# Two routed expert layers: gates gathered as a column of the rows, results scaled as they leave PSUM, choices combined by one addition, last block stored by halves

## The reference

```python
# 1. local attention: each token is a softmax-weighted sum of itself and 6 before it
out = np.einsum('bshk,bskhg->bshg', softmax(weight_gen), x_unf)     # 8 heads, 7 taps

# 2. first expert layer, two of eight experts per token
noisy = x @ w_gate + np.log1p(np.exp(x @ w_noise)) * noise
top2_w = softmax of the two largest
out[mask] += top2_w[mask, k, None] * (np.maximum(x[mask] @ w1[e], 0.0) @ w2[e])

# 3. second expert layer, one of eight
logits = (x / (|x| + 1e-6)) @ (emb / (|emb| + 1e-6)).T / tau
gate_w = softmax(logits) at the argmax
out[mask] = gate_w[mask, None] * (np.maximum(x[mask] @ v1[e], 0.0) @ v2[e])
```

## Time and profile before

| | us |
|---|---|
| runs, median (lowest to highest) | 1224.87 (1224.33 to 1225.34) |
| profiled execution, its own time | 1223.82 |
| its span | 1222.1 |
| PE busy | 1095.9 (90%) |
| DVE busy | 744.1 (61%) |
| ACT busy | 553.1 (45%) |
| POOL busy | 523.2 (43%) |

### The profile page before, as it was taken

The page is one execution under the profiler, slowest core; times in us unless marked ns, Lnnn a source line. Parts: engine busy times, 40 slices in busy tenths (PEclk is TensorE's granted clock), DMA queues, the critical chain, the costliest instruction groups (busy, mean ns, idle before and its releaser), DMA issues.

```text
span 1222.1 us, 27227 instructions
## 1 busy us (share of the span) xinstructions
PE 1095.9 (90%) x8052; PEld 1039.5 (85%) x8052; DVE 744.1 (61%) x1406; ACT 553.1 (45%) x1552; POOL 523.2 (43%) x639
## 2 busy tenths in 40 slices
PE   1989188999999999999999999786389999999997
PEld 0556176999999999999999999765279999999997
DVE  8998795446464644646455465386854664466663
ACT  2222285445454544545444454355644554455552
POOL 5887002444444444444444444400324444444444
PEclk9999589999999999999999999988589999999999
DMA  9111201213131121313113111182622313124521
GB/s 325 70 63 52 73 1 42 77 42 99 39 101 42 55 83 40 98 40 101 43 39 93 39 41 41 38 268 92 240 62 64 98 42 100 39 65 125 138 61 35
DMA packets 51188, 97.89 MB, mean 80 GB/s; under 512 B 9651, under 2 KB 33051, under 8 KB 50876
## 3 DMA queue, kind: packets, MB, share of 16 engines
q1 hardware_dynamic: 33084, 61.77, 16.7%
q0 software_dynamic: 18048, 35.42, 10.1%
HBM read 69.62 MB, written 29.10 MB: 81 GB/s over the span
## 4 chain that ended last, share of the span: by engine, by line
PE 78%; DVE 12%; issue 3%; POOL 3%; ACT 2%; DMA 2%; DVEq 0%; POOLq 0%; ACTq 0%; SPq 0%
PE banks L624 22%; PE banks L626 11%; PE banks L610 9%; PE banks L616 7%; PE banks L615 7%; PE banks L611 7%; PE banks L612 7%; DVE prods L889 3%; POOL prods L443 2%; PE banks L586 2%; PE banks L594 2%; PE banks L595 2%; PE banks L550 1%; DVE choices L1092 1%; PE banks L540 1%
## 5 line engine op out<-in xcount | busy, mean ns | idle before, releaser
L1050 DVE SCALAR_TENSOR_TENSOR h_lo<-banks,h_hi 128x256 fp32r<-128x256 f32 x736 | 312.1, 424 | 372.4 <-ACT h_hi L774 315.0
L774 ACT ACTIVATE h_hi<-banks 128x256 fp32r<-128x256 f32 x736 | 283.3, 385 | 448.7 <-PE banks L616 347.6
L624 PE MATMUL banks<-w_hl,h_hi 128*128 128x384 f32 x1472 | 466.0, 353 | 0.0
L626 PE MATMUL banks<-w_hl,h_lo 128*128 128x192 f32 x1472 | 371.1, 252 | 0.0
L626 PEld LDWEIGHTS banks<-w_hl,h_lo 128*128 128x128 f32 x1472 | 279.6, 190 | 0.0
L624 PEld LDWEIGHTS banks<-w_hl,h_hi 128*128 128x128 f32 x1472 | 276.0, 188 | 0.4
L451 POOL DMA_INDIRECT x_slots<-token_rows,gather_idx x192 | 192.4, 1002 | 105.4 <-POOL gather_idx L448 76.2
L610 PE MATMUL banks<-x_hi_a,w_hi 128*128 (+1 forms) x736 | 225.0, 306 | 1.8 <-DVE x_hl_b L1018 1.7
L611 PE MATMUL banks<-x_hi_a,w_lo 128*128 (+1 forms) x736 | 206.5, 281 | 0.0
L616 PE MATMUL banks<-x_hl_b,w_lo 128*128 (+1 forms) x736 | 206.3, 280 | 0.0
L615 PE MATMUL banks<-x_hl_b,w_hi 128*128 (+1 forms) x736 | 205.8, 280 | 0.0
(11 more groups left out here) (170 smaller groups left out, 1255.3 us busy)
## 6 DMA issues: line engine op xcount, KB each, us to landing
raw<-in_moe_w SPq DMA_DIRECT2D x17, 768.0 KB
choices<-choice_rows SPq DMA_DIRECT2D x28, 384.0 KB, 4.2
raw<-in_moe_w SPq DMA_DIRECT2D x17, 512.0 KB
raw<-in_moe_w SPq DMA_DIRECT2D x34, 256.0 KB
x_halo<-in_x SPq DMA_DIRECT2D x2, 2688.0 KB, 15.1
token_rows<-stage SPq DMA_DIRECT2D x14, 384.0 KB, 2.3
token_rows<-rows SPq DMA_DIRECT2D x14, 384.0 KB, 3.9
x_slots<-token_rows,gather_idx POOLq DMA_INDIRECT x192
```

The costliest lines, as they stand in the source:

```text
L624: mm(y[:, i, 0:2 * D], h_hi[:, c % HBUFS, t], w2_hl[u][:, c, :, :], start=c == 0, stop=False)
L626: ins = mm(y[:, i, 0:D], h_lo[:, c % HBUFS, t], w2_hl[u][:, c, 0, :], start=False, stop=c == FC - 1)
L774: sc.activation(h_hi[:, c % HBUFS, :], banks[:, c % HBANKS, 0:BLOCK], ACT.Relu).then_inc(h_hi_ready[m], 1)
L1050: v.scalar_tensor_tensor(h_lo[:, c % HBUFS, :], banks[:, c % HBANKS, 0:BLOCK], 0.0, h_hi[:, c % HBUFS, :].bitcast(F32), ALU.max, ALU.subtr ...
```

## The change

- Rows in DRAM are 193 long (`ROW`); the last value is the gate. `token_rows[0]` now has a copy per choice (14336 rows), so each attention group is stored twice, and `choice_rows` is unchanged. `store_gates` writes the column: four DMAs of 3584 values in the first layer (two choices, two batches), two in the second, each value 4 bytes at a step of 772. The first gather waits for them.
- POOL takes the gates of a block out of the gathered rows to a ring of four (`take_gates`); ACT scales one half of the results by them (`take_half`), DVE multiplies and adds the other (`add_half`), each in two pieces.
- The combination is one addition per group. The rows of the second layer are stored unscaled, after all choices have been loaded. No `keep_clock` per group; 26 idle matmuls ahead of the groups in place of 9, not waiting for the first choice. There are two buffers of turned rows.
- The second router picks on raw scores; 1/tau is in the embeddings, and the norm enters only in the gate. Gates are computed partly while PE ranks, partly before the fourth group of hots. The block table is written after the hots; `positions` is shorter; indices of the first layer point into the doubled rows directly.
- In the last block POOL copies the indices ahead, PE signals the first half (`half_done`), and each half is scaled, added and stored by itself.

```diff
 SP
+                for k in range(CHOICES[0]):
+                    sp.dma_start(token_view(token_rows[0][k * N:(k + 1) * N])[b, :, jj * GROUP:(jj + 1) * GROUP, 0:D],
+                                 stage[g % 2][:]).then_inc(rows_stored[g % 2], 16)
+            def store_gates(m):
+                for k in range(CHOICES[m]):
+                    for b in range(B):
+                        sp.dma_start(token_view(token_rows[m][k * N:(k + 1) * N])[b, :, :, D:D + 1],
+                                     gate[k][:, b * J:(b + 1) * J].unsqueeze(2), allow_slow_non_contiguous=True).then_inc(gates_stored[m], 16)
+            sp.wait_ge(weights_ready, 1)
+            load_expert(w1, w2, 1)
+            sp.wait_ge(gates_ready[0], 1)
+            store_gates(0)
+            with sp.Fori(2, E) as e:
...
+            for g in range(NG):
+                b, jj = divmod(g, GB)
+                sp.wait_ge(rows_ready[1], g + 1)
+                sp.dma_start(token_view(token_rows[1])[b, :, jj * GROUP:(jj + 1) * GROUP, 0:D],
+                             rows[:, g * GROUP:(g + 1) * GROUP, :]).then_inc(x1_stored, 16)
+            sp.wait_ge(gates_ready[1], 1)
+            store_gates(1)
 POOL
+                def take_gates(n):
+                    at = n % RING * HALVES
+                    gp.tensor_copy(gate_ring[:, bass.ds(at if isinstance(n, int) else pool.snap(at), HALVES)].unsqueeze(2),
+                                   x_slots[:, :, D:D + 1]).then_inc(gates_taken[m], 1)
...
                     pool.wait_ge(x_turned[m], g + 3)
+                    take_gates(g + 2)
                     gather(g + 3)
+                    pool.wait_ge(gates_taken[m], g + 3)
...
+                    if last:
+                        pool.wait_ge(stored[m], g * 32)
+                        copy_idx()
+                        pool.wait_ge(idx_copied[m], g * 2 + 4)
+                        pool.wait_ge(half_ready[m], 1)
+                        store_half(0)
+                        pool.wait_ge(y_ready[m], g + 3)
+                        store_half(1)
+                        return
-            for g in range(SCALE_ACT, NG):
-                tiles = slice(g * GROUP, (g + 1) * GROUP)
-                gp.tensor_tensor(rows[:, tiles, :], rows[:, tiles, :],
-                                 gate[0][:, tiles].unsqueeze(2).to_broadcast([P, GROUP, D]), ALU.mult).then_inc(pool_gated, 1)
+            mixture(1, out, N - 1, [(x1_stored, 16 * NG), (gates_stored[1], 16 * B)])
 PE
+                        if last and i == 0:
+                            ins.then_inc(half_done[m], 1)
-            pe.wait_ge(choices_in[0][0], 16)
-            keep_clock(9)
+            keep_clock(26)
-                keep_clock(4)
 ACT
-                    sc.copy(y_half(parity(act, g)), y[:, :, D:2 * D]).then_inc(y_copied[m], 1)
+                    if last and i == 0:
+                        act.wait_ge(half_done[m], 1)
+                    else:
+                        act.wait_ge(h_used[m], g * FC + (FC + HBUFS))
+                    sc.activation(y_half(parity(act, g), i), y[:, i, D:2 * D], ACT.Copy,
+                                  scale=slot_gate(act, g, i)).then_inc(y_copied[m], 1)
-            sc.sqrt(table_probe[:], ident[:, 0:1])
-            with act.Fori(0, SCALE_ACT) as g:
...
 DVE
+                step(v.tensor_tensor_scan(cum[:, 1:], flat, flat, 0.0, ALU.add, ALU.max))
+                first_of_expert, last_of_expert = cum[:, 0:E * T:T], cum[:, T::T]
+                step(v.tensor_tensor(totals[:], last_of_expert, first_of_expert, ALU.subtract))
...
+                    if g == HOT_BUFS:
+                        finish_gates()
...
+                block_table()
                 v.memset(gather_rows[:, cols:cols + AHEAD], 0)
                 dve.wait_ge(hots_used[m], n // ONEHOTS)
...
-                    v.tensor_tensor(slots, y[:, :, 0:D], slots, ALU.add).then_inc(y_ready[m], 1)
+                    ins = v.scalar_tensor_tensor(slots, y[:, i, 0:D], slot_gate(dve, g, i), slots, ALU.mult, ALU.add)
+            for g in range(NG):
+                dve.wait_ge(choices_in[g % CHOICE_BUFS], g // CHOICE_BUFS * 32 + 32)
+                first, second = (choices[g % CHOICE_BUFS][:, k, :].rearrange("p (i d) -> p i d", d=D) for k in range(2))
+                v.tensor_tensor(rows[:, g * GROUP:(g + 1) * GROUP, :], first, second, ALU.add).then_inc(rows_ready[1], 1)
+            def weigh_best():
+                dve.wait_ge(roots_ready, 1)
+                step(v.tensor_scalar(inv_norm[:], inv_norm[:], 1e-6, None, ALU.add))
+                step(v.reciprocal(inv_norm[:], inv_norm[:]))
+                step(v.tensor_tensor(r["noisy"][:], scores, best[0][:].unsqueeze(2).to_broadcast([P, T, E]), ALU.subtract))
+                v.tensor_tensor(r["noisy"][:], r["noisy"][:], inv_norm[:].unsqueeze(2).to_broadcast([P, T, E]),
+                                ALU.mult).then_inc(route_ask[1], 1)
```

More of the change, by code:

```diff
@@ L397, in _ @@
             gp.memset(ident[:], 0.0).then_inc(consts_step, 1)
-            gp.memset(before[:], 1.0).then_inc(consts_step, 1)
+            gp.memset(not_after[:], 0.0).then_inc(consts_step, 1)
             gp.memset(ones[:], 1.0)
@@ L838, in _ @@
             sc.activation(r["noisy"][:], r["noisy"][:], ACT.Exp).then_inc(route_act[1], 1)
-            act.wait_ge(route_ask[1], 2)
-            with act.Fori(0, SCALE_ACT) as g:
-                for i in range(GROUP):
-                    tile = rows[:, bass.ds(g * GROUP + i, 1), :].rearrange("p o d -> p (o d)")
-                    ins = sc.activation(tile, tile, ACT.Copy, scale=gate[0][:, bass.ds(g * GROUP + i, 1)])
-                ins.then_inc(gated, 1)
             hot_rows(1)
@@ L922, in _ @@
             finish_rows(NG - 1)
+            v.memset(cum[:, 0:1], 0.0)
+            step(v.memset(block_end[:, 0:1], 0.0))
             def pick(k, scores):
```

240 lines of the change are left out of this document (119 added, 121 removed).

## The result

The changed kernel takes 1212.58 us (median of 5 runs, 1212.21 to 1213.03), the kernel before 1225.34 beside it (5 runs, 1224.33 to 1226.58): a ratio of 0.9895 [0.9881, 0.9908]. It is 12.8 us faster, where 32.9 were forecast. The profiled execution took 1213.03, its span is 1211.2 (before 1222.1).

A forecast was written before the change was run, and what follows sets the result against it. TensorE bounds the expert blocks; only the mostly-DVE stretches between could shrink. 3.5 + 4.0 + 17.6 + 9.1 - 1.3 = 32.9 us off 1223.82, plus 1.05 for the median, gives 1192; range 1186 to 1198, with rivals 1184 to 1213.

The forecast's parts named there:

- Combination: Adding the two choices, up to the second routing's maximum: 19.6 us earlier, 17.6 without the 2.0 counted at the last block.
- TensorE takes the bound, 2.40: Combination, per group: six transposes 0.99 plus twelve products 1.41 make TensorE the limit, 2.40 us for each of 14 groups.
- Rival 2: Combination: TensorE's clock drops without the clock-keeping matmuls, 3.0 us a group, 1200 in all; chance 0.12, shared with Rival 4.
- The last block: End of each mixture: storing by halves, with indices copied ahead, ends 2.0 us earlier, twice, 4.0 in all.
- the sign: End of the program: the last store would begin about 2.1 us after ACT starts on the last results, 4.1 before.
- The gate column: Both routings: 4-byte gate writes to DRAM stay hidden before the gather, with 36 and 29 ns a write available; zero cost.
- end long before the gather: Second routing: stores of the rows, 5.4 MB, follow the last choice load and finish well ahead of the gather.
- Second routing: From the maximum to POOL's index copy: 32.5 us in place of 41.6, 9.1 less.
- Rival 4: Second routing: small steps stay slow although POOL is idle, 7 us, 1199 in all; chance 0.12, shared with Rival 2.
- First routing: First layer's routing: shorter DVE gate, count and id steps, less gate steps in the hots loop, net 3.5 us earlier.
- Inside the blocks: Expert blocks: extra gate copies and split ACT and DVE steps mostly hidden behind TensorE, 1.3 us lost in all.
- Rival 3: Gate column: 4-byte writes go out one behind another, 1279 at 98.7 ns each, whole gain gone at 58; chance 0.11.

The follow-up runs named there:

- e6: e1 with two clock-keeping matmuls per combination group in place of four; 1199.95 us.
- e1: Changed kernel with the combination's clock-keeping matmuls put back, nine once the first choices have landed and four per group; 1201.44 us.
- e3: Kernel before the change, with only the four clock-keeping matmuls per combination group taken out; 1231.03 us.
- e2: Changed kernel with twenty more clock-keeping matmuls behind the wait for the first choices, none in the groups; 1212.35 us.
- e8: Changed kernel with each mixture's last block back in its old order, waiting for both halves before the stores; 1214.48 us.
- e4: Changed kernel with POOL's copy of the last block's store indices moved ahead of its wait for the previous block's stores; 1211.28 us.
- e10: e6 with the second mixture's table at a row pitch of 832 bytes in place of 772; 1192.07 us.
- e9: e6 with the second mixture's rows widened by POOL and stored in one piece by SP; 1201.51 us.
- e7: Changed kernel with every gate column stored four times, three to unread spare tensors, gathers waiting for all; 1294.63 us.
- e11: e9 with e4's order and 24 in place of 10 clock-keeping matmuls ahead of both mixtures' first turns; 1201.20 us.
- e12: e10 with e4's order and 20 in place of 10 clock-keeping matmuls ahead of the first mixture's first turn; 1190.69 us.

## Why the prediction was wrong

- **Combination, the failed step.** "TensorE takes the bound, 2.40": the two terms, 0.99 and 1.41, were read at a granted clock of 1.00, which the four matmuls held that the same edit removes. Measured without them: 3.73 at 0.50 (2.01 at 1.00 in e6), so the maximum at 849.83 and not 831.5; 19.0 of the 22.0 us missing in the profile. Rival 2 named the mechanism, but with too small a price and too small a chance. It scaled the group by one row, the six transposes of 1.23 in the earlier trace rows, as if they had run at the low clock; the clock rose while they ran (0.50 up to 800.4, 0.82 from there to 801). Wholly at 0.50 six take 1.55, and the group's transposes and products together take nearly twice as long (2.01 to 3.73). And its "against" was wrong: that TensorE was busy all the time did not keep the clock. e1 and e3 show that the matmuls do it, e2 that a warm start does not. The bound itself, 2.40, was too high by the overlap of 0.39; that made no difference here, and helped e6 to look right. The Trainium skill ("TensorE: Matmul & The Clock Gate", Part 4: PE-mode transpose) says that the full clock does not engage for transposes; here transposes and products ran in turn, and the last 24 products by themselves were granted 0.50 as well, so it is not the transposes alone; no run says what either does without the other over a longer stretch.
- **The last block, mis-sized.** 2.0 a mixture was expected, 0.7 measured; from ACT's start to the last store it is 3.6, where 2.1 was to be the sign. The halves themselves were sized rightly (0.73 and 0.77 for two of 0.35 each), and the second store follows the first by 1.28, as the working had it. What it put at next to nothing is the passing from engine to engine. The first store was to begin 1.1 behind TensorE's end and begins 2.5 behind: ACT starts 0.13 behind (0.40 in e8, so half_done is worth 0.3), DVE 0.90 behind ACT, the store 1.44 behind DVE (1.22 in e4, with the indices ahead), and of all this the first half's own work is only some 0.75.
- **The gate column, right here, and for too simple a reason.** 36 and 29 ns a write were at hand, 23.8 and 25.1 were needed, and both index copies wait for DVE. But that the stores of rows "end long before the gather" held only because the combination was slow: at a pitch of 772 bytes they move 152 GB/s and not the 396 of before. They push the column 4.5 us past the routing as soon as the combination is as fast as predicted (e6), and at a pitch of 832 bytes they do not (e10).
- **Second routing, right.** 32.5 forecast, 32.49 measured; the gates were asked for 17.2 behind the maximum (17.1 in the working). Rival 4 falls: the steps are back at 0.17 as POOL is idle, and e9, where POOL works beside DVE, shows two larger steps at about double their time.
- **First routing, right.** 3.5 forecast, 3.76 measured. Attention ended 1.6 later in this profile; in e1, e2 and e4, which have the same attention, member starts at 139.17, 138.49 and 139.51, so these 1.6 are not shown to be an effect of the change.
- **Inside the blocks, right.** TensorE at 99.9 to 100, and the second layer's stretch from first product to last is 314.0 for 313.7. One small loss was not foreseen. The ten clock-keeping matmuls ahead of the first gather, moved in front of the register loads, now end at 192.4, the first transposes wait until 195.3 and find the clock down (0.48 for the first of them, 0.33 before), and the first product comes 7.5 behind the index copy where it came 7.0.
- Rival 3, slower, falls: even at 24 ns a write the column is hidden; it would have needed 58.

With the clock kept and the rows aligned (e10), the kernel takes 1192.07, the 1192 of the prediction. Part of that agreement is luck: the last blocks still give less, the combination takes 42.6 and not 40.9, and the first layer's blocks took 2 us less in e10 than in e6.

## What to carry to other kernels

A duration read from a trace holds only at the clock of its window: before removing matmuls that do nothing, ask what holds the clock without them, and price the stretch at both levels, product by product. Take a group's price from the starts of one group and the next, not from the sum of busy times, which overlap. When the slowest step of a stage is made faster, look again at every transfer that it had been hiding, and test the fast version and not only the change as it stands. A table in DRAM whose rows get one word longer can lose more than the word: here the stores of its rows fell to less than half their rate, and a pitch of 832 bytes, 13 x 64, the only other one tried, brought most of it back.

## What the runs showed of the hardware

- TensorE busy for 10.00 of 10 us can be granted 0.50. Two clock-keeping matmuls per group held 1.00 in the profile of e6, and its other four runs took the same time; with one, times went from 1198.7 to 1214.7 from run to run.
- A store of 768-byte rows moves 152 GB/s at a pitch of 772 bytes (e6) and 325 at 832 (e10); pieces of 3088 bytes at the pitch of 772 move 368 (e9).
- Strided writes of 4 bytes to DRAM cost a DMA engine 24 to 25 ns each, issue and landing included, for 1792 as for 3584 of them (e7).
- Beside a POOL copy of 128 x 768 numbers, DVE steps over two operands take 1.13 to 1.27 for 0.62; a cast 0.90 for 0.39; a reduction beside it kept its 0.62 (e9 against e10).
- Not settled: the stretch from the first index copy to the first load of choices, with the same code for the blocks, took 599.4 in e6, 601.5 in e9, 601.2 in e11, 597.5 in e10 and 596.6 in e12. These kernels differ in where their tiles and instructions lie; no run separates the two.
